# A slot matrix's products ahead of the preceding expert's subtraction, in three pairs of accumulator banks, and the class counts' products last

## The reference

```
out = np.einsum('hk,bskhg->bshg', w, x_unf)          # seven taps, softmax weights
x = out.reshape(B * S, D)
# soft mixture: 32 slots, 8 experts of 4
logits = x @ phi
slot_input = softmax(logits, axis=0).T @ x
slot_out[e] = np.maximum(slot_input[e] @ w1[e], 0.0) @ w2[e]
x = softmax(logits, axis=1) @ slot_out               # = c @ slot_out
# top-2 mixture
noisy_logits = x @ w_gate + np.log1p(np.exp(x @ w_noise)) * noise
top2 = np.argpartition(-noisy_logits, 2, axis=1)[:, :2]
out[mask] += top2_w[mask, k, None] * (np.maximum(x[mask] @ w1[e], 0.0) @ w2[e])
```

## Time and profile before

| what | us |
|---|---|
| runs of the kernel before | 1028.18, 1023.93, 1034.09; median 1028.18 |
| the profiled execution, time | 1030.94 |
| its span on the core | 1029.2 |
| TensorE busy in it | 948.9 (92%) |
| the slot matrices' loop on TensorE, first product to last subtraction | 314.66 to 359.68 |
| VectorE's wait for the summed counts | 6.30 |

### The profile page before, as it was taken

How to read it: one execution, slowest core, us unless ns; L and a number is a source line. 1 busy time by engine, 2 the same in 40 slices (tenths; PEclk the granted TensorE clock), 3 DMA queues, 4 the chain that set the end, 5 groups by cost and what they waited for, 6 DMA issues and landing times.

```text
span 1029.2 us, 25913 instructions
## 1 busy us (share of the span) xinstructions
PE 948.9 (92%) x7871; PEld 738.0 (72%) x7872; DVE 636.2 (62%) x1363; ACT 462.6 (45%) x975; POOL 343.5 (33%) x358
## 2 busy tenths in 40 slices
PE   6999989988888747899999999999999999999995
PEld 5999989971364323677877777777777777777774
DVE  3223442445227797788876776767767677776773
ACT  2222212211013424555555665656556565665663
POOL 4000000010000021334445454555545666666652
PEclk9999989998997959899999999999999999999998
DMA  7465965654642410333333333333334444444441
GB/s 227 123 201 168 243 217 184 220 178 129 180 120 79 108 70 14 96 92 97 93 105 109 108 108 107 115 107 109 111 103 116 105 110 112 107 109 106 115 112 38
DMA packets 75148, 127.49 MB, mean 124 GB/s; under 512 B 10541, under 2 KB 43773, under 8 KB 73177
## 3 DMA queue, kind: packets, MB, share of 16 engines
q1 hardware_dynamic: 58936, 108.78, 35.5%
q0 software_dynamic: 15248, 17.49, 8.2%
q10 hardware_dynamic: 912, 0.52, 0.2%
HBM read 63.49 MB, written 16.86 MB: 78 GB/s over the span
## 4 chain that ended last, share of the span: by engine, by line
PE 84%; DVE 5%; DMA 5%; issue 2%; ACT 2%; another core or an unknown queue 0%; POOL 0%; SPq 0%; DVEq 0%; PEldq 0%; ACTq 0%; POOLq 0%
PE ps L1373 29%; PE ps L1377 15%; PE ps L1352 10%; PE ps L1136 9%; DMA stage<-in_moe_w 4%; PE ps L1185 3%; PE ps L1187 3%; PE ps L1129 3%; PE ps L1291 3%; PE ps L1327 2%; PE ps L1217 2%; PE ps L1342 1%; PE ps L1244 1%; PE ps L1274 1%; PE ps L1406 1%
## 5 line engine op out<-in xcount | busy, mean ns | idle before, releaser
L620 ACT ACTIVATE x_ring<-ps 128x512 f16<-128x512 f32 x472 | 256.4, 598 | 211.8 <-PE ps L1352 178.5
L1373 PE MATMUL ps<-w2hl,x_ring 128*128 x1888 | 346.9, 327 | 1.4 <-DVE x_ring L1080 0.7
L1070 DVE SCALAR_TENSOR_TENSOR x_ring<-ps,x_ring 128x512 f16<-128x512 f32 x472 | 302.9, 683 | 9.8 <-ACT x_ring L620 3.1
L1373 PEld LDWEIGHTS ps<-w2hl,x_ring 128*128 128x128 f16 x1888 | 176.4, 97 | 97.4 <-issue 7.4
L495 POOL DMA_INDIRECT stage<-pay_rows,row_id x151 | 150.4, 996 | 259.6 <-PE ps L1352 160.8
L1377 PE MATMUL ps<-w2hl,x_ring 128*128 x1888 | 194.4, 246 | 1.1 <-DVE x_ring L1070 1.1
L505 POOL DMA_INDIRECT out_rows<-x_ring,row_id x151 | 170.2, 1127 | 59.8 <-issue 45.3
L1377 PEld LDWEIGHTS ps<-w2hl,x_ring 128*128 128x128 f16 x1888 | 162.9, 98 | 32.1 <-DVE x_ring L1070 1.9
L1352 PE MATMUL ps<-c,x_ring 96*128 96x128 f16 x1888 | 145.4, 220 | 2.3 <-DVE c L1063 2.3
L1063 DVE COPY c<-ps 96x256 f16<-96x256 f16 (+1 forms) x151 | 38.9, 258 | 145.3 <-PE ps L1342 123.5
L1352 PEld LDWEIGHTS ps<-c,x_ring 96*128 96x128 f16 x1888 | 122.5, 98 | 2.8 <-issue 2.7
(11 more groups left out here) (279 smaller groups left out, 707.3 us busy)
## 6 DMA issues: line engine op xcount, KB each, us to landing
x_ring<-a SPq DMA_DIRECT2D x236, 192.0 KB
stage<-in_moe_w SPq DMA_DIRECT2D x48, 768.0 KB, 8.0
x_ring<-in_x SPq DMA_DIRECT2D x14, 1536.0 KB, 7.1
stage<-pay_rows,row_id POOLq DMA_INDIRECT x151
out_rows<-x_ring,row_id POOLq DMA_INDIRECT x151
pay_rows<-x_ring SPq DMA_DIRECT2D x1, 1904.0 KB, 6.0
gbuf<-in_moe_noise ACTq DMA_DIRECT2D x1, 448.0 KB, 4.9
x_halo<-in_x SPq DMA_DIRECT2D x4, 72.0 KB, 3.9
```

The lines of the kernel that those rows point to most:

```text
L620: a.activation(hh[:, m % 2, 4 * half:4 * half + 4, :].rearrange("p j q -> p (j q)"), ps[:, 2 + 2 * (m % 2) + half, :], ACT.Relu).then_inc( ...
L1070: last = v.scalar_tensor_tensor(hl[:, m % 2, 4 * half:4 * half + 4, :].rearrange("p j q -> p (j q)"), ps[:, 2 + 2 * (m % 2) + half, :], 0. ...
L1373: t_.matmul(ps[:, 6 + b % 2, 0:2 * D], hh[:, m % 2, j, :], w, start=k == 0 and j == 0, stop=False)
```

## The change

Three things change. On TensorE the subtraction of expert `e - 1` (`less_high`) now stands behind the products of expert `e`. Three pairs of banks (0 to 5) take turns in place of two, so that the products of `e` need the low part of `e - 3` to be copied and not that of `e - 2`. ScalarE's two copies are split accordingly: `a_high(e)`, then `a_low(e - 1)`; the exponential of the gates (`m_exp`) stands ahead of the last expert's `a_high`, as it did. And the two products that sum the class counts leave the place ahead of the last expert: they now come after the last subtraction, in bank 6, since bank 4 belongs to the third pair. The weights still have two places, and SyncE's program is the same.

```diff
             def a_high(e):
                 act.wait_ge(a_ps, e + 1)
-                a.activation(a3[:, e, :], ps[0:KS, 2 * (e % 2):2 * (e % 2) + 2, :].rearrange("p a f -> p (a f)"),
+                a.activation(a3[:, e, :], ps[0:KS, 2 * (e % 3):2 * (e % 3) + 2, :].rearrange("p a f -> p (a f)"),
                              ACT.Copy).then_inc(a_hi, 1)
+
+            def a_low(e):
                 act.wait_ge(a_sub, e + 1)
...
-            for e in range(E - 1):
+            a_high(0)
+            for e in range(1, E):
                 a_high(e)
-            act.wait_ge(m_diff, 1)
-            a.activation(gm[:, 2, :], gm[:, 2, :], ACT.Exp).then_inc(m_exp, 1)
-            a_high(E - 1)
+                a_low(e - 1)
+                if e == E - 2:
+                    act.wait_ge(m_diff, 1)
+                    a.activation(gm[:, 2, :], gm[:, 2, :], ACT.Exp).then_inc(m_exp, 1)
+            a_low(E - 1)
...
-            step(v.tensor_copy(cnt[:, 1:3, :].rearrange("p a e -> p (a e)"), ps[:, 4, 0:2 * NCL]))
+            step(v.tensor_copy(cnt[:, 1:3, :].rearrange("p a e -> p (a e)"), ps[:, 6, 0:2 * NCL]))
...
+            def less_high(e):
+
+                pe.wait_ge(a_hi, e + 1)
+                for half in range(2):
+                    mm = t_.matmul(ps[0:KS, 2 * (e % 3) + half, :], low_only[:, :],
+                                   a3[:, e, half * BANK:(half + 1) * BANK], start=False, stop=True,
+                                   skip_group_check=True)
+                mm.then_inc(a_sub, 1)
             for e in range(E):
                 n = 2 * E + e
-                if e == E - 1:
-
-                    pe.wait_ge(cnt_ready, 1)
-                    t_.matmul(ps[:, 4, 0:NCL], tri[:, :], cnt[:, 0, :], start=True, stop=True)
-                    t_.matmul(ps[:, 4, NCL:2 * NCL], ones[:, :], cnt[:, 0, :], start=True, stop=True
-                              ).then_inc(off_ps, 1)
                 pe.wait_ge(w1s_in[n % 2], 16 * (n // 2 + 1))
-                if e >= 2:
-                    pe.wait_ge(a_lo, e - 1)
+                if e >= 3:
+                    pe.wait_ge(a_lo, e - 2)
...
                 mm.then_inc(a_ps, 1)
-                pe.wait_ge(a_hi, e + 1)
...
-                mm.then_inc(a_sub, 1)
+                if e:
+                    less_high(e - 1)
+            less_high(E - 1)
+            pe.wait_ge(gl_evac, QGROUPS)
+            pe.wait_ge(cnt_ready, 1)
+            t_.matmul(ps[:, 6, 0:NCL], tri[:, :], cnt[:, 0, :], start=True, stop=True)
+            t_.matmul(ps[:, 6, NCL:2 * NCL], ones[:, :], cnt[:, 0, :], start=True, stop=True).then_inc(off_ps, 1)
```

More of the change, by code:

```diff
@@ L587, in a_high @@
                 act.wait_ge(a_ps, e + 1)
-                a.activation(a3[:, e, :], ps[0:KS, 2 * (e % 2):2 * (e % 2) + 2, :].rearrange("p a f -> p (a f)"),
+                a.activation(a3[:, e, :], ps[0:KS, 2 * (e % 3):2 * (e % 3) + 2, :].rearrange("p a f -> p (a f)"),
                              ACT.Copy).then_inc(a_hi, 1)
+            def a_low(e):
                 act.wait_ge(a_sub, e + 1)
-                a.activation(a3[NS:2 * NS, e, :], ps[NS:2 * NS, 2 * (e % 2):2 * (e % 2) + 2, :].rearrange(
+                a.activation(a3[NS:2 * NS, e, :], ps[NS:2 * NS, 2 * (e % 3):2 * (e % 3) + 2, :].rearrange(
                     "p a f -> p (a f)"), ACT.Copy).then_inc(a_lo, 1)
@@ L1277, in _ @@
             pe.wait_ge(s3_ready, 1)
+            def less_high(e):
[5 more added lines that the diff above has]
+                mm.then_inc(a_sub, 1)
             for e in range(E):
                 n = 2 * E + e
-                if e == E - 1:
-                    pe.wait_ge(cnt_ready, 1)
-                    t_.matmul(ps[:, 4, 0:NCL], tri[:, :], cnt[:, 0, :], start=True, stop=True)
-                    t_.matmul(ps[:, 4, NCL:2 * NCL], ones[:, :], cnt[:, 0, :], start=True, stop=True
-                              ).then_inc(off_ps, 1)
                 pe.wait_ge(w1s_in[n % 2], 16 * (n // 2 + 1))
-                if e >= 2:
-                    pe.wait_ge(a_lo, e - 1)
+                if e >= 3:
+                    pe.wait_ge(a_lo, e - 2)
                 for half in range(2):
                     for c in range(2):
-                        mm = t_.matmul(ps[0:KS, 2 * (e % 2) + half, :],
+                        mm = t_.matmul(ps[0:KS, 2 * (e % 3) + half, :],
                                        slot_s3[:, c, :, :].rearrange("p r s -> p (r s)"),
```

## The result

| | us |
|---|---|
| the kernel before, median of 20 runs | 1031.55 |
| the changed kernel, median of 20 runs | 1034.69 |
| ratio, 95% interval | 1.0036, 1.0021 to 1.0051 |
| the profiled execution, time and span | 1035.29, 1033.5 |

The change makes the kernel **0.36% slower** (3.7 us by the ratio, which goes by all runs; interval 2.2 to 5.3; the medians lie 3.1 us apart), where 0.3 us was forecast with a range up to 1033.5. Of the 6.2 us between the forecast 1028.5 and the median, 3.4 are the kernel before itself: over 20 runs its median is 1031.55, not the 1028.18 of the three runs shown. Four more sets of times, taken with the experiments on four chips, gave the change 1.0028, 1.0021, 1.0004 and 1.0010. Weighted by their intervals, the five make 1.0022 with about 0.0008 to either side: **2.3 us**, against 0.3.

What follows compares the result with a forecast made beforehand. The counts' products' start bounds the stage; transfers take over the loop. 7.6 us of waits go, 2.8 return, the eighth expert adds 5.2: 0.3 us later, median 1028.5 us, no change; range 1024 to 1033.5.

Steps and rivals of the forecast that it cites:

- What bounds the loop: Expert loop: weight transfers take over from the waits for ScalarE, since any turn over 4.53 us exceeds TensorE's 8.16.
- The sum: Up to the counts: 7.6 us of waits go, 2.8 come back, the eighth expert adds 5.2; 0.3 us later.
- 338.00 + 3T: Time in us at which the counts' products start after the change; 354.38 forecast, against 354.09 before.
- T: Turn from one expert's products' end until those two experts later can start: landing plus 0.06 us; 5.46, bounds 4.86 to 5.86.
- The eighth expert's 5.17 us: End of the loop: the counts now follow the eighth expert, which adds 4.08 + 1.09 = 5.2 us ahead of them.
- TensorE's own period: Expert loop: TensorE's work per expert without waits, 3.45 + 0.63 = 4.08 us.
- rival A: Expert loop: TensorE stays the bound, turn under 4.53 us, counts 2.5 us earlier, 1025.7 us; chance 12%.
- the granted clock: Expert loop: idle time per expert falls from 1.09 us to about half, so nothing added for TensorE's clock level.
- The turns: Expert loop: three rounds of two experts, each T + 3.63 us, 0.93 longer than TensorE's work, bring 2.8 us back.
- theory N: From the experiments' expectations, not the prediction: the rest of the loss is spread from stages ahead of the loop.
- Rival B: Weight transfers slow each other down; at T = 9.36 counts 12.0 us later, 1040.2 us; chance 4% for over 1% slower.
- Rival C: Start of the blocks: the stretch at the lower clock becomes longer, 5 us at most; chance 3%.

Runs made afterwards that it cites:

- the filled form: The changed kernel plus four unused float16 products ahead of the third, fifth and seventh expert's products; 0.9995 and 1.0005 of the kernel before, weighted 1.0002.

## Why the prediction was wrong

- **What bounds the loop: right.** The transfers took over (the third, fifth and seventh expert's products waited 1.84, 1.06 and 0.67 us for them, where 0.9 to 1.5 was forecast), the waits for ScalarE went from 8.9 us to 0.7, the counts came last and VectorE waited 6.5 us.
- **The sum: right where the clock held.** 338.00 + 3T gives 1.2 us at the first profile's landings, measured 1.1; the second, with T at 5.49 by its landings of 5.00, 5.56 and 5.72, gives 0.4, measured 0.3. I took T = 5.46; the two have 5.75 and 5.49. The eighth expert's 5.17 us measured 5.2. TensorE's own period was 3.86 and not 4.08, which matters only without waits: rival A's gain would have been 4.4, not 2.5 us.
- **The step that failed is the granted clock,** put at nothing with "the idle time per expert falls". The sum of the idle time was the wrong thing to look at. The old order spreads it in pauses of 1.1 us; the new one works through two groups and then pauses 1.2 to 3.0 us at once, and in four of six profiles the third expert's products then ran at the lower level for 1.7 to 3.4 us more. That term is worth 1.7 to 4.1 us where it comes (2.4 to 4.8 less the 0.7 of the profiles without it; the longer waits of the third and sixth are in it), about 1.9 over the six, and the forecast had zero. The turns, at 0.7 us in the profiles without a fall, are near the forecast 0.3. That the fall costs this much in the loop is read off the profiles; the times agree with it in size, but theory N above isn't excluded as a part of them.
- **The row that said so was there.** I took the soft mixture's first layer as the model of a transfer-bound loop and read its waits, but chose the rows of four starts that ran at the upper level, and read from them that every expert's products start from a wait; in that profile five of eight do. The group just ahead of them holds two experts' products, 16 MATMULs behind a pause of 1.96 us, and took more than twice 3.62 us, since the clock had fallen. Its row, and the stretch in it (columns as in the earlier trace rows):

```profile
241.57 8.75 PE L1217 MATMUL ps<-stage,x_ring 96*32 96x512 f32 x16 [1.96 <-DMA stage<-in_moe_w]
...
242.20:245.60 3.40, 3.40 (x5) 0.71 (x4) 3.33 (x3) 0.00 (x0) 0.00 (x0) 0.50 0.53 125
```

The changed kernel's profile of that same layer shows it twice:

```profile
242.26 8.75 PE L1222 MATMUL ps<-stage,x_ring 96*32 96x512 f32 x16 [2.17 <-DMA stage<-in_moe_w]
252.95 10.36 PE L1222 MATMUL ps<-stage,x_ring 96*32 96x512 f32 x16 [1.94 <-DMA stage<-in_moe_w]
```

- **Rival A** was wrong: the 36 transfers of the six profiles landed in 4.8 to 6.8 us. The Trainium skill ("DMA: Bandwidth & Descriptors", Anatomy of one DMA — SWDGE (gpsimd) path) fits a transfer that GpSimd issues with 2.0 us plus its bytes at 436 GB/s, an estimated 3.8 us for 768 KB. SyncE issues these, and none of them came near it. **Rival B**, transfers slowed by each other, did not come: a period of 4.7 us left the landings at 4.8 to 5.9 us but for two, 6.81 and 6.14 us in the third and sixth profile, both for the third expert, whose cause is open. They cost more through the clock than by themselves. **Rival C**, the clock at the blocks' start, is there with some 0.7 us.
- **The level of the range** hung on three runs; the median over 20 lay 3.4 us higher. Within this range an unchanged kernel would have been near its upper end.

What stays open: the five sets of times lie between 0.4 and 3.7 us, and the profiles tell of six executions only; with the two of the experiments the clock fell in five of eight. That the filled form wins this back is shown in its profiles and by all sets together, not by times on the same chip. How much of the times comes from ahead of the loop (theory N) is not known, nor why the first set says 3.7 us where its own profile's loop lost 1.1.

## What to carry to other kernels

Moving a wait away from one releaser exposes the next. Compute the next loop (place free, transfer, work) before the edit: here two places gave 5.7 + 3.7 us per two experts, and the reordering bought less than it moved. A short dependent result on which another engine waits must not stand behind bulk work: placing two small products one expert later cost 5.7 us, and placing them one expert earlier, with the class starts' transposes, won 4.3, as much as the reordering of all the bulk with the counts left in place (5.3 by its times, 3.2 in its profile). And ask how long the longest single pause of TensorE becomes, not only how much it idles in sum.

## What the hardware showed that was not expected

- Eight of these float32 products take 3.60 us when run on and 3.67 from a wait at the upper level, 5.37 to 7.05 us after a pause of 1.6 to 3.0 us in four of six executions of the change; in the other two, with pauses of 1.2 and 1.8 us, the clock held.
- The same transfer of 768 KB, with no other large transfer in flight than one more like it for a part of the time, landed between 4.8 and 6.8 us.
- 38 unused products at the start of the blocks, 8.5 us of TensorE's time, made the kernel before 2.6 us faster (0.5 to 4.6). In its profile the first blocks then run at the upper level, and are through 1.2 to 1.6 us sooner after the lookups than in the second and third profile of the kernel before.
